# Attention, FFT mixing, FFN and a gated convolution in one kernel: probabilities times values per head, accumulators opened by transposes

## The reference, cut to what matters

```python
mask = q_bucket[:, :, :, None] == k_bucket[:, :, None, :]      # 6 sign bits of q @ proj, k @ proj
scores = np.where(mask, scale * (q @ k.T), -1e9)
attn = exp(scores - max) / (sum + 1e-9)
x = (attn @ v) laid out as (B, S, H * D)

mixed = np.real(fft(fft(x, axis=1), axis=2))
u = x + mixed
un = (u - mean(u)) / sqrt(var(u) + 1e-6)
x = u + relu(un @ w_ch1) @ w_ch2

gate = sigmoid(causal_conv5(x, conv_w))
out = (gate * (x @ w_val)) @ w_out
```

## Time and profile before

| | |
|---|---|
| time, median of 3 runs | 663.28 us (663.13 to 665.55) |
| the profiled execution | 663.62 us, span 661.8 us |
| PE busy | 634.2 us (96%), 3810 instructions |
| PEld busy | 508.4 us (77%) |
| DVE busy | 353.8 us (53%) |
| ACT busy | 317.0 us (48%) |
| POOL busy | 245.4 us (37%) |
| mean DMA rate | 64 GB/s |
| granted TensorE clock | 0.9 or more in each fortieth of the span |

### The profile page before, as it was taken

The page is one execution under the profiler, slowest core; times in us unless marked ns, Lnnn a source line. Parts: engine busy times, 40 slices in busy tenths (PEclk is TensorE's granted clock), DMA queues, the critical chain, the costliest instruction groups (busy, mean ns, idle before and its releaser), DMA issues.

```text
span 661.8 us, 11290 instructions
## 1 busy us (share of the span) xinstructions
PE 634.2 (96%) x3810; PEld 508.4 (77%) x3810; DVE 353.8 (53%) x585; ACT 317.0 (48%) x606; POOL 245.4 (37%) x201
## 2 busy tenths in 40 slices
PE   2999999999999999889999999999999999999998
PEld 1667676767666675888888888889888888888786
DVE  2978786968787785987211111115433333329920
ACT  2877776868686765364322222224333333255242
POOL 6643333333252440845333222235544444313140
PEclk9999999999999999999999999999999999999999
DMA  5922231314241000100122222431212222000102
GB/s 127 247 77 72 72 95 48 95 48 108 59 119 57 15 25 1 49 0 1 33 65 63 63 63 63 141 115 33 63 63 63 63 63 63 16 1 1 64 32 95
DMA packets 34263, 42.08 MB, mean 64 GB/s; under 512 B 3521, under 2 KB 22209, under 8 KB 34241
## 3 DMA queue, kind: packets, MB, share of 16 engines
q1 hardware_dynamic: 32512, 37.77, 19.7%
q0 software_dynamic: 1728, 4.02, 2.3%
HBM read 38.63 MB, written 3.15 MB: 63 GB/s over the span
## 4 chain that ended last, share of the span: by engine, by line
PE 84%; DVE 8%; issue 3%; POOL 2%; ACT 1%; DMA 1%; SPq 0%; DVEq 0%; ACTq 0%
PE banks L1516 20%; PE banks L1504 20%; PE banks L1319 10%; PE banks L1302 10%; PE banks L1366 7%; PE banks L1595 4%; PE banks L1611 4%; DVE row_min L970 2%; PE banks L1258 2%; PE banks L1439 2%; PE banks L1491 1%; DVE probT L342 1%; DVE k_b L963 1%; PE banks L1342 1%; POOL row_sums_and_differences L540 1%
## 5 line engine op out<-in xcount | busy, mean ns | idle before, releaser
L1165 DVE SCALAR_TENSOR_TENSOR h_lo<-banks,h_hi 128x512 fp32r<-128x512 f32 x64 | 35.5, 558 | 186.4 <-ACT h_hi L826 186.4
L970 DVE TENSOR_REDUCE row_min<-banks 128x1 f32<-128x768 f32 x96 | 91.3, 956 | 44.3 <-PE banks L1302 43.8
L677 ACT ACTIVATE prob<-banks,row_min 128x768 f32<-128x768 f32 x96 | 87.0, 906 | 30.1 <-DVE row_min L970 30.1
L1504 PE MATMUL banks<-unT_hi,w_hi 128*128 128x512 f32 (+1 forms) x256 | 86.5, 338 | 0.0
L1504 PE MATMUL banks<-unT_hi,w_lo 128*128 128x512 f32 (+1 forms) x256 | 86.3, 337 | 0.0
L1504 PE MATMUL banks<-unT_lo,w_hi 128*128 128x512 f32 (+1 forms) x256 | 86.2, 337 | 0.0
L1366 PE MATMUL banks<-ident,prob 128*128 128x128 f32 x576 | 79.7, 274 | 2.2 <-DVE probT L342 1.2
L563 POOL TENSOR_TENSOR w_lo<-w_stage,w_hi 128x512 fp32r<-128x512 f32 x32 | 45.1, 1411 | 83.2 <-ACT w_hi L742 83.2
L1366 PEld LDWEIGHTS banks<-ident,prob 128*128 128x128 f32 x576 | 67.2, 140 | 10.2 <-ACT probT L342 2.6
L501 POOL TENSOR_TENSOR k_b<-k_raw,k_a 64x768 fp32r<-64x768 f32 x16 | 29.2, 1823 | 123.2 <-ACT k_a L660 123.2
L1319 PE MATMUL banks<-probT,v_in 128*64 128x384 f32 x384 | 72.3, 498 | 0.7 <-ACT outT L687 0.7
(11 more groups left out here) (149 smaller groups left out, 1204.1 us busy)
## 6 DMA issues: line engine op xcount, KB each, us to landing
w_stage<-in_moe_w_ch SPq DMA_DIRECT2D x64, 256.0 KB, 2.8
q_raw<-in_q SPq DMA_DIRECT2D x32, 192.0 KB, 3.3
k_raw<-in_k SPq DMA_DIRECT2D x32, 192.0 KB, 3.6
v_in<-in_v SPq DMA_DIRECT2D x16, 192.0 KB, 2.4
out<-y_out SPq DMA_DIRECT2D x12, 256.0 KB, 2.0
seq_tables_sb<-in_dft POOLq DMA_DIRECT2D x6, 386.0 KB, 3.6
wvo_stage<-in_moe_w_val SPq DMA_DIRECT2D x1, 1024.0 KB, 5.4
wvo_stage<-in_moe_w_out SPq DMA_DIRECT2D x1, 1024.0 KB, 7.9
```

The source lines that it names most:

```text
L677: act.activation(prob[s % 2][:, :, :], s_tile(s), ACT.Exp, bias=row_min[:, s:s + 1], scale=-1.0, accum_out=row_sum[:, s:s + 1]).then_inc(e ...
L970: dve.tensor_reduce(row_min[:, s:s + 1], s_tile(s), AX.XY, ALU.min).then_inc(min_ready, 1)
L1165: dve.scalar_tensor_tensor(out=h_lo[:, slot, at:at + size], in0=h_bank[c], scalar=0.0, in1=h_hi[:, slot, at:at + size].bitcast(F32), op0=A ...
L1504: op = pe.matmul(h_bank[c], w_[:, slot, kb, :], x_[:, kb, at:at + size], start=(kb == 0 and m == 0), stop=(kb == KB - 1 and m == 2))
```

## The change

Four things change together.

1. The product of probabilities and values is made per head. For each of 6 key tiles the two matmuls side by side are the two query halves of one head, with the same values. A head's 12 matmuls are two parts of six; the four parts of a pair stand in slot 9 of the pair and slots 0, 3 and 6 of the next. O moves from slots 3 and 6 to slots 5 and 11, `copy_outT` from 1 and 4 to 1 and 7, the sums are inverted per head in slots 8 and 2 (10 and 1 before), and X is written per head. v is loaded per head, and the loop begins at pair 2, with pair 1 written out.
2. `open_acc` uses transposes (`is_transpose=True`) of the six tiles in the order in which they are stored; the `reverse` matrix goes. A block takes 6 instructions.
3. `unT_hi` and `unT_lo` keep the folded order, one copy for each tile.
4. `take_x2` restores the natural order: four copies for each block, one of a single column and two that read PSUM backwards.

```diff
-        OUT_SLOT = {3: 0, 6: 1}
+        OUT_SLOT = {5: 0, 11: 1}
-        PV_SLOTS = {11: (0, 0), 0: (0, 1), 1: (0, 2), 2: (1, 0), 3: (1, 1), 4: (1, 2)}
+        PV_PARTS = 2
+        PV_SLOTS = {9: (0, 0, 0), 0: (1, 0, 1), 3: (1, 1, 0), 6: (1, 1, 1)}
...
-            def load_v(i):
-
-                need(sp, pv_done, 2 * i)
-                for h in range(2):
-                    sp.dma_start(v_in[:, h, :, :], v_v[2 * i + h]).then_inc(v_loaded, 16)
+            def load_v(i, h):
+
+                need(sp, pv_done, 2 * i + (h - 1) if not isinstance(i, int) or i else 0)
+                sp.dma_start(v_in[:, h, :, :], v_v[2 * i + h]).then_inc(v_loaded[h], 16)
...
-                for kt in (2 * part, 2 * part + 1):
-                    for h in range(2):
-                        op = pe.matmul(PS[h * D:(h + 1) * D, 7, 0:HALF], v_in[:, h, kt, :],
+                for kt in range(T // PV_PARTS * part, T // PV_PARTS * (part + 1)):
+                    for g in range(2):
+                        op = pe.matmul(PS[g * D:(g + 1) * D, 7, 0:HALF], v_in[:, h, kt, :],
                                        probT[h][:, kt, g * HALF:(g + 1) * HALF], start=(kt == 0), stop=(kt == T - 1))
...
-                    if s == 10 and last < 2:
+                    if s == 8 and last < 2:
                         invert_sums(i, 0)
-                    if s == 1 and not first:
+                    if s == 2 and not first:
                         invert_sums(i - 1, 1)
...
-                for t in range(T):
-                    for rows, cols in natural(t):
...
-                        pe.matmul(acc(d, c)[:, left - low:right - low], X[:, b, t, d * P:(d + 1) * P],
-                                  mover[:, at:at + right - left], start=first, stop=False, skip_group_check=True)
-                        first = False
+                tiles = (range(C0 // P), range(C0 // P, T))[c]
+                for t in tiles:
+                    at = t * P - c * C0
+                    pe.matmul(acc(d, c)[:, at:at + P], X[:, b, t, d * P:(d + 1) * P], ident[:, :], is_transpose=True,
+                              start=(t == tiles[0] and (c == 0 or d % 2 == 0)), stop=False, skip_group_check=True)
...
-                    act.copy(half[:, 0:C0 - HALF], PS[:, d, HALF:C0]).then_inc(x2_by_act, 1)
-                    act.copy(half[:, C0 - HALF:HALF], acc(d, 1)).then_inc(x2_by_act, 1)
+                    act.copy(half[:, 0:1], PS[:, d, HALF:HALF + 1]).then_inc(x2_by_act, 1)
+                    act.copy(half[:, C1 + 1:HALF], PS[:, d, C0 - 1:HALF:-1]).then_inc(x2_by_act, 1)
+                    act.copy(half[:, C1:0:-1], acc(d, 1)).then_inc(x2_by_act, 1)
```

More of the change, by code:

```diff
@@ L175, in attention_fft_ffn_gate_kernel @@
         qk_loaded = [sem(f"qk_loaded{h}") for h in range(2)]
-        v_loaded = sem("v_loaded")
+        v_loaded = [sem(f"v_loaded{h}") for h in range(2)]
         scratch_full = [sem(f"scratch_full{r}") for r in range(3)]
@@ L266, in attention_fft_ffn_gate_kernel @@
             counts[-1, (0, task)] = count[n % 3]
-        for i in (0, NP - 1, NP):
+        for i in (0, 1, NP - 1, NP):
             if i == NP - 1:
-                after_first = list(count)
-                count = [c + per * (NP - 2) for c, per in zip(count, PER)]
+                after_second = list(count)
+                count = [c + per * (NP - 3) for c, per in zip(count, PER)]
             for use in uses:
@@ L335, in drain_prob @@
             wait_filled(eng, i, use)
-            if h == 0 and qt % HT == 0:
-                need(eng, pv_done, pair_ * 2 + (qt // HT - 1))
+            if qt == 0:
+                need(eng, pv_done, pair_ * 2 + (h - 1))
             half = int(task[1])
@@ L428, in _ @@
             load_qk(0, 1)
-            load_v(0)
+            load_v(0, 0)
+            load_v(0, 1)
             load_qk(1, 0)
@@ L725, in pair @@
                         copy_outT(i, 0)
-                    if s == 4 and not (isinstance(i, int) and i == 0):
+                    if s == 7 and not (isinstance(i, int) and i == 0):
                         copy_outT(i, 1)
+                    if last == 2 and s in (2, 3):
+                        round_parts(0, s - 2)
             round_k(0, 0)
@@ L732, in _ @@
             pair(0, 0)
-            with act.Fori(1, NP - 1) as i:
+            pair(1, 0)
+            with act.Fori(2, NP - 1) as i:
                 pair(i, 0)
@@ L757, in unT_hi @@
                 src = PS[:, un_bank(n), :].rearrange("p (k m) -> p k m", k=KB)
-                for rows, cols in natural(t):
-                    act.copy(un_hi[b][:, :, cols], src[:, :, rows]).then_inc(unT_hi_done, 1)
+                act.copy(un_hi[b][:, :, t * P:(t + 1) * P], src).then_inc(unT_hi_done, 1)
             def normalise(n):
@@ L1044, in _ @@
             pair(0, 0)
-            with dve.Fori(1, NP - 1) as i:
+            pair(1, 0)
+            with dve.Fori(2, NP - 1) as i:
                 pair(i, 0)
@@ L1378, in pair @@
                     if s in PV_SLOTS:
-                        g, part = PV_SLOTS[s]
-                        if s == SLOTS - 1:
-                            if last < 2:
-                                p_times_v(i, g, part)
-                        elif not first:
-                            p_times_v(i - 1, g, part)
-            pe.wait_ge(consts_ready, 9)
+                        back, h, part = PV_SLOTS[s]
+                        if not back and last < 2:
+                            p_times_v(i, h, part)
+                        if back and not first:
+                            p_times_v(i - 1, h, part)
+            pe.wait_ge(consts_ready, 7)
             pe.wait_ge(w_ready, 2)
@@ L1391, in _ @@
             pair(0, 0)
-            with pe.Fori(1, NP - 1) as i:
+            pair(1, 0)
+            with pe.Fori(2, NP - 1) as i:
                 pair(i, 0)
@@ L1410, in transpose_un @@
                 if before is not None:
-                    pe.wait_ge(unT_lo_done, unT_pieces(before))
+                    pe.wait_ge(unT_lo_done, before + 1)
                 for kb in range(KB):
```

141 lines of the change are left out of this document (57 added, 84 removed).

## The result

The changed kernel takes 665.92 us (median of 20 runs, 664.18 to 667.02), the kernel before in the same session 663.39 us (20 runs, 662.81 to 666.10). The ratio is 1.0027, 95% interval [1.0017, 1.0038]: 1.8 us slower, within the 0.5% that the prediction counts as no change. (The means differ by 1.8 us, the medians by 2.5: the runs of each kernel lie in two clusters, see the end of the part on why the prediction was right.) Its profiled execution took 664.56 us, its span is 662.9 (before: 663.62 and 661.8), so the profile shows +1.1. (The pair from 100.78 that the rows of before call pair 2 is pair 3 when the first is counted as 0. Pairs are counted from 0 here.)

What follows compares the result with a forecast made beforehand. TensorE was taken to bound the attention pair (busy 30.20 of 30.68 us). Attention +5.6, second opening -4.0, first -1.5 and copies +0.2 gave 663.9, or 663.6 us against the runs' median; range 656.5 to 668.

Steps and rivals of the forecast that it cites:

- the class: No change, within 0.5% (3.3 us), chance 0.52; faster than 660 and slower than 666.6 had 0.24 each.
- the two large terms: Attention +5.6 us against openings -4.0 and -1.5: two changes of some 5 us that cancel.
- A: TensorE's own work in a steady pair: from 29.6 to 29.3 us, 0.3 gained by four groups of six matmuls.
- B: Waits inside a pair: 0.69 us before outT transposes in slots 5 and 11, 0.58 in slot 0; 1.96 against 1.10.
- The 0.58 in slot 0: Bank waits at the pair's wrap: 0.33 us at slot 0's first probability transposes, 0.25 at its second.
- my adders: TensorE time per slot: 1.38 us, plus 2.26 per group of six, 0.96 bits, 0.27 bucket matmul, 0.36 outT transpose.
- C: First and last pairs of attention: +0.4 us at pair 0, +1.8 at pair 7; with pairs 1 to 6, attention +5.6.
- D: Accumulator openings after attention, by transposes: second batch -4.0 us, first -1.5, small copies +0.2.
- rival 2: An opening transpose costs 0.22 us, like the fp32 matmul, or the clock falls: 667.1 us; chance 0.10.
- Rival 1: DVE frees the bank in time, so the pair's waits vanish: pair 29.3 to 29.5, 650 to 652 us; chance 0.14.
- Rival 3: DVE falls further behind, invert_sums standing behind two bucket compares: seven pairs lose 0.6 us more each, 667.8; chance 0.12.
- Rival 4: One head's two halves don't run side by side: +1.9 us for each of 32 groups, 60 us; chance 0.02.

Runs made afterwards that it cites:

- kb_short: Changed kernel with DVE's compare for k_b's second half over 8 columns in place of 384 in pairs 2 to 6, mask partly uncomputed; 661.38 us, 0.9949.
- pv_three: Changed kernel with each head's values in three groups of four matmuls in place of two of six; 654.13 us, 0.9849 against the kernel before.
- open_twice: Changed kernel with each of the four openings of batch 0's first 512 columns issued twice (16 more transposes); 664.92 us, 1.0011 against the kernel before.
- attn_only: Kernel before with only the changed attention (values per head, groups of six), openings still by matmuls; 670.09 us, 1.0086.
- open_only: Kernel before with only the openings by transposes, u and x2 in plain tile order; 659.28 us, 0.9915.
- pv_mixed: Kernel with three groups per head, with head 0 back in two groups of six, one head 1 group and outT copy moved; 652.03 us, 0.9802 against before.

## Why the prediction was right

The time (663.6 for 665.9) and the class were right, and the two large terms were, each by its own mechanism.

- **A, the work.** TensorE busy 29.67 us in a pair where I had 29.3; groups of 2.16 us by the timeline. Right in sign (0.53 gained for 0.3).
- **B, the two waits.** Written as 0.69 and 0.69, released by k_b; measured 0.70 and 0.61, released by k_b, and kb_short shows that they follow the length of that compare one to one. None in slots 9 and 10, right. The 0.58 in slot 0 was right in size and in kind, but in the loop it is hard to see: there slot 0 takes only 0.1 more than slot 6 (3.73 against 3.63), and 0.45 stand ahead of it, in the gap at the turn, which I had not thought of. Where the loop ends there is no gap, slot 0 takes 4.17, 0.52 to 0.54 more than slot 6, and the wait ahead of its transposes is released by DVE's copy of probT, as written. They start 5.30 us after slot 10's scores, and I had 5.21. In pv_three the same wait shows, smaller: the probability transposes of slot 0 take 1.13 us where others take 0.82, and slot 0 takes 3.28 for slot 6's 2.98. What I left out is that slots 5 and 11 lose more than the wait itself: slot 5 is 0.9 us longer than the same slot without a wait (2.64 against 1.71 in pv_three). By the slots' lengths all of this makes 0.25 us more of waits than the 1.96 I wrote, and the other slots take 0.25 less than my adders, slots 3 and 9 above all; that the pair came out at 31.31 for 31.26 is in part luck.
- **C, first and last pairs.** This is the term that was mis-sized: attention costs +6.5 for +5.6, and the miss lies in pairs 0 and 1. +0.93 by the start of pair 1 for +0.4: 0.25 by the first scores, and the wait for k_b takes 0.66. The 0.25 need not be the change's, for the first scores start between 14.48 and 14.80 in the thirteen traces; the rest is, for up to slot 5 pair 0 takes 11.8 us in both. (In other traces these six slots, with the same work, take 11.5 to 12.8 us, so pair 0 is a poor place to compare kernels.) Pair 1 lost 1.14 for 0.57. TensorE's timeline at its start:

```profile
40.37 0.59 PE L1288 MATMUL banks<-k_a,q_a 128*128 128x384 f32 x2 [0.66 <-DVE k_b L950]
...
41.87 0.84 PE L1352 MATMUL banks<-ident,prob 128*128 128x128 f32 x6 [0.56 <-DVE probT L342]
```

Here the bank wait of slot 0 that B foresaw does stand, 0.56 us, for pair 0 has no outT transposes that would hold TensorE back first. Pair 7 +1.75 for +1.8; pairs 2 to 6 +2.85 for +2.85.
- **D, the openings.** Second: 4.1 (4.0). First: 1.2 without the clock's fall and 1.0 with it, for 1.5; I had taken 0.4 for the openings between the waits, and these wait for ACT's tiles (0.95 us twice), which may hold more of that back; no run separates it. A transpose that opens a sum costs 0.109 us, as a plain one: rival 2 is out. The Trainium skill ("TensorE: Matmul & The Clock Gate", Part 4) says that transposes don't count as busy for the clock gate in the way matmuls do. The traces don't bear that out: the clock stays at 1.00 in the run of 24 in each of the eleven traces that have it, and sixteen more transposes in the first openings kept it up (open_twice).
- **Rival 1** (the waits vanish, 650 to 652) had a chance of 0.14. As a forecast of the changed kernel it is out. As a statement of what the pair's work is worth it was near: pv_three's pair is 29.8.
- **Rival 3** (DVE falls behind further): not seen; the waits are those of B.
- **Rival 4** (the two halves of a head don't run side by side): out, a group of twelve takes 2.16 us.

By the profiles the sum is +1.1 for +0.3. The median is 2.3 us above the forecast; the other part of that is which cluster the medians fall in. The runs of the changed kernel fall into two clusters (9 of 664.2 to 665.1, 11 of 665.6 to 667.0), those of before too (14 of 662.8 to 664.0, 6 of 664.5 to 666.1). The mean granted clock, on record for each run on the four chips of the experiments, tells the clusters of before apart without an exception: 33 runs with 0.999 or more take 662.58 to 664.45 us, 28 runs with 0.997 take 664.51 to 666.11, and the medians are 1.7 us apart. In the changed kernel the lower cluster has 1.0 or 0.997, and the upper 0.997 or 0.995; its profiled execution is of the lower one and has the fall in the first openings, which costs 0.2. So in before a fall of the clock goes with the upper cluster; where it lies in the runs that weren't profiled isn't shown, nor what decides whether it comes.

Left open: why the two parts together cost 1.8 us [1.1, 2.5] where their sum is about 0 (plus or minus 1.4). Runs with a clock of 0.999 or more bring the two nearer: attn_only +5.8 and open_only -5.3, the latter from a single run. The spans of the profiles agree (+6.0 - 3.0 with open_only's clock fall of 1.1 and first pair of 0.9, which makes +1.0, for +1.1).

## What to carry to other kernels

Read a rotation of banks by who drains each one and what stands in that engine's queue: the wait that counts is the queue's length, and moving the waiting instruction to another bank mostly moves the wait. A longer group of matmuls saves a switch, but it gathers cover in one slot and takes it from the ones behind it; here four groups of six cost 1.5 us a pair more than six groups of four, and with one head's three groups of four made into two of six, in slots with room, the pair was 0.3 shorter. When two parts of a change cancel, run them apart: the good part alone was worth 5.6 us, and with the bad part mended the kernel gained another 4.4 us (pv_three, an edit of two lines) to 7.5 (pv_mixed). And before a gap is charged as a cost, look at what stands behind it: the gap at the loop's turn, 0.45 us a pair, only took the place of a wait.

## What the runs showed of the hardware that I had not expected

- At the turn of the loop TensorE started the next scores 0.24 us after outT transposes that had not waited (pv_three), and 0.87 us after ones that had just waited, where 0.42 to 0.44 us stand between the same instructions elsewhere (after, slot 5 and the end of the loop). Why isn't shown. It cost nothing here: the slots on both sides together take 6.73 us where the loop turns and 6.74 where it ends.
- The granted clock fell to 1.2 GHz for some 3.5 us behind stretches with waits in them (TensorE busy 1.69 us of 3 in after, 1.20 of 2 in open_only). In the first openings, with waiting transposes, the stretch was 0.2 us longer with the fall in after and 0.9 in kb_short; in the matmuls ahead of them it was some 1.1 longer. Where it falls differs between profiled executions whose waits are the same (1.72 us ahead of the feature products in open_only, with a fall, and in the changed kernel, without). A repeat of four openings, which leaves the sums as they are, held it up in the profile and in 9 of 12 runs at no cost.
- An fp32 transpose of 128x128 that opens a sum, to which the next matmuls add, takes 0.109 us, half of the two records of the fp32 matmul with an identity (0.11 each).
